# Router gates of tiles 0 to 7 as row sums on VectorE instead of turned rows and small matmuls on TensorE

## The reference, cut to what matters

```python
# _moe_ref: x is the attention output, (4, 576, 512)
u = x + real(fft(fft(x, axis=1), axis=2))
un = (u - mean(u)) / sqrt(var(u) + 1e-6)
x2 = u + maximum(un @ w_ch1, 0) @ w_ch2          # 512 -> 2048 -> 512
# _moe2_ref: 8 experts, 512 -> 1024 -> 512
logits = x2 @ w_gate                             # (512, 8)
local_gate = sigmoid(x2 @ w_local)               # (512, 1)
# position s takes argmax(logits) if s == 0 or local_gate < 0.5, else the expert of position s - 1
out[s] = softmax(logits)[e] * (maximum(x2[s] @ w1[e], 0) @ w2[e])
```

## Time and profile before

| | |
|---|---|
| median of 3 runs | 913.07 us (912.81 to 913.15) |
| the profiled execution, its own time | 915.11 us |
| its span, first to last instruction | 913.3 us |
| mean granted TensorE clock | 0.976 of full speed |
| TensorE busy | 859.9 us, 94% |
| VectorE busy | 460.6 us, 50% |
| ScalarE busy | 316.1 us, 35% |
| GpSimd busy | 272.5 us, 30% |

### The profile page before, as it was taken

One profiled execution on the slowest core, in us unless ns is written; L12 is line 12 of the kernel. 1 busy time (PEld: TensorE's weight loads), 2 busy tenths in 40 slices (PEclk: granted clock), 3 DMA queues, 4 the chain that ended last, 5 costly groups with the idle time before them and its releaser, 6 DMA issues.

```text
span 913.3 us, 22516 instructions
## 1 busy us (share of the span) xinstructions
PE 859.9 (94%) x9075; PEld 622.1 (68%) x9076; DVE 460.6 (50%) x852; ACT 316.1 (35%) x469; POOL 272.5 (30%) x287
## 2 busy tenths in 40 slices
PE   8988988899999999999999999929999999999995
PEld 4766767776767676767676767617777777777773
DVE  6889898857242424242424244658995884000000
ACT  5788887643111111111111111111333333333331
POOL 2457768311010101010101000002444444343331
PEclk9999999989999999999999999968999999999998
DMA  9454652455010101010101003504775772111110
GB/s 287 128 172 143 183 142 72 146 181 162 24 48 23 46 23 46 23 46 23 46 23 46 24 24 106 148 26 125 244 232 159 233 233 94 46 42 45 50 29 1
DMA packets 55675, 88.92 MB, mean 97 GB/s; under 512 B 7148, under 2 KB 26171, under 8 KB 55621
## 3 DMA queue, kind: packets, MB, share of 16 engines
q1 hardware_dynamic: 50261, 72.43, 25.7%
q0 software_dynamic: 5360, 15.74, 5.6%
HBM read 70.80 MB, written 16.55 MB: 96 GB/s over the span
## 4 chain that ended last, share of the span: by engine, by line
PE 77%; DVE 9%; DMA 5%; issue 3%; ACT 2%; SPq 2%; POOL 1%; DVEq 0%; POOLq 0%; ACTq 0%
PE psum L925 19%; PE psum L908 19%; PE psum L1089 14%; PE psum L1105 14%; DMA m_mem<-in_qk 2%; PE psum L660 2%; DVE m_mem L1416 1%; DMA arena<-in_mlp_w 1%; PE psum L1056 1%; DVE arena L1444 1%; PE psum L869 1%; DVE arena L1437 1%; DVE arena L1465 1%; PE psum L877 1%; PE psum L773 1%
## 5 line engine op out<-in xcount | busy, mean ns | idle before, releaser
L908 PE MATMUL psum<-m_mem,arena 128*128 (+1 forms) x1728 | 199.0, 273 | 0.0
L925 PE MATMUL psum<-arena,m_mem 128*128 128x512 f16 x864 | 195.3, 379 | 0.0
L908 PEld LDWEIGHTS psum<-m_mem,arena 128*128 128x128 f16 x1728 | 168.5, 98 | 25.9 <-issue 0.4
L925 PEld LDWEIGHTS psum<-arena,m_mem 128*128 128x128 f16 x864 | 84.5, 98 | 90.4
L1089 PEld LDWEIGHTS psum<-m_mem,arena 128*128 x2400 | 137.1, 97 | 7.0 <-issue 1.5
L1089 PE MATMUL psum<-m_mem,arena 128*128 128x128 f16 x2400 | 139.4, 218 | 1.3 <-issue 0.7
L1105 PE MATMUL psum<-arena,m_mem 128*128 x600 | 133.4, 379 | 0.0
L1272 ACT ACTIVATE m_mem<-psum 128x512 f16<-128x512 f32 x72 | 42.9, 596 | 242.4 <-PE psum L908 242.4
L1105 PEld LDWEIGHTS psum<-arena,m_mem 128*128 128x128 f16 x600 | 57.7, 98 | 65.2
L1598 DVE SCALAR_TENSOR_TENSOR m_mem<-psum,m_mem 128x512 f16<-128x512 f32 x72 | 49.7, 690 | 100.0 <-ACT m_mem L1272 99.9
L1994 POOL TENSOR_TENSOR arena<-m_mem,arena 128x1024 f16<-128x1024 f32 x9 | 18.0, 1996 | 270.1 <-ACT arena L1287 225.1
(11 more groups left out here) (242 smaller groups left out, 1071.7 us busy)
## 6 DMA issues: line engine op xcount, KB each, us to landing
dimdft_sb<-in_exp_w SPq DMA_DIRECT2D x74, 256.0 KB, 3.6
wstage<-in_exp_w SPq DMA_DIRECT2D x54, 256.0 KB, 3.0
m_mem<-in_qk SPq DMA_DIRECT2D x16, 576.0 KB, 4.8
arena<-in_v SPq DMA_DIRECT2D x32, 160.0 KB, 2.8
x_rows<-m_mem SPq DMA_DIRECT2D x16, 320.0 KB, 3.0
x_rows<-arena SPq DMA_DIRECT2D x9, 512.0 KB, 2.8
wstage<-in_mlp_w SPq DMA_DIRECT2D x16, 256.0 KB, 3.2
arena<-in_mlp_w SPq DMA_DIRECT2D x16, 256.0 KB, 3.6
```

Of the source, the lines that this page charges most:

```text
L908: last = nc.tensor.matmul(psum[:, 2 + k % 4, (f % 2) * 2 * P:(f % 2 + 1) * 2 * P], w1_sb[:, sp_, c, f * P:(f + 1) * P], unT[:, bass.ds(t % ...
L925: last = nc.tensor.matmul(psum[:, 6 + q, :], hT[:, k % 4, sp_, at:at + P], w2_sb[:, mp, f, :], start=f == 0 and sp_ == 0 and mp == 0, stop ...
```

## The change

The rows of x2 are not turned for tiles 0 to 7. For each of the nine gate columns and each half q, VectorE multiplies the 128x512 rows elementwise by the column, laid out as a row and repeated on all 128 partitions, and sums the products over the row into one word of `logits` per partition (`scalar_tensor_tensor` with an accumulator output). These are 18 instructions per tile, three behind `hidden_lo(0)` and five behind each of `hidden_lo(1)` to `hidden_lo(3)` of the following tile. The products themselves are written to a scratch space and not used.

The repeated columns are made ahead of tile 0: TensorE transposes the 128x36 gate matrix, VectorE copies it out, SyncE stores its 36 rows to memory and, behind the last MLP weight load, issues nine DMAs that read each column as a repeated source into 128 partitions (256 KB each). The last tile (t = 8) keeps the turned rows and the matmuls. The waits of `x2_of` and of the routing stage are changed to the new semaphore `gate_step`.

The diff, without its context lines:

```diff
@@ -120,6 +120,7 @@
+    gate_dram = nc.dram_tensor("gate_rows", [DC * (E + 1), P], F32).ap()
@@ -282,6 +283,12 @@
+        gate_at = [SLOT_WORDS, SLOT_WORDS + 2 * D] + [SLOT_WORDS - 2 * D * (i + 1) for i in range(5)]\
+            + [x_tail + 4 * D, x_tail + 6 * D]
+        gate_cols = [arena[:, at:at + 2 * D].bitcast(F32) for at in gate_at]
+        gateT = arena[0:DC * (E + 1), ends_at + 4 * D - 2 * P:ends_at + 4 * D].bitcast(F32)
+        assert ends_at + 4 * D <= min(gate_at)
+        products = [x288.bitcast(F16)[:, i * D:(i + 1) * D] for i in range(2)]
@@ -448,9 +455,11 @@
-        x2T_ready = sem("x2T_ready")
-        x2T_hi = sem("x2T_hi")
-        x2T_lo = sem("x2T_lo")
+        gateT_ready = sem("gateT_ready")
+        gateT_copied = sem("gateT_copied")
+        gate_out = sem("gate_out")
+        gate_in = sem("gate_in")
+        gate_step = sem("gate_step")
@@ -609,8 +618,15 @@
+            sp.wait_ge(gateT_copied, 1)
+            sp.dma_start(gate_dram, gateT).then_inc(gate_out, 16)
+            sp.wait_ge(gate_out, 16)
+            for e in range(E + 1):
+                sp.dma_start(gate_cols[e].rearrange("p (c j) -> p c j", c=DC),
+                             gate_dram.rearrange("(c e) j -> e c j", c=DC)[e].unsqueeze(0).to_broadcast([P, DC, P]))\
+                    .then_inc(gate_in, 16)
@@ -870,14 +886,6 @@
-            def transpose_x2(t):
-                pe.wait_ge(x2_done, t + 1)
-                for q in range(2):
-                    for c in range(DC):
-                        last = nc.tensor.transpose(psum[:, q, c * P:(c + 1) * P], x2_sb[:, q, c * P:(c + 1) * P],
-                                                   ident_sb[:, :])
-                last.then_inc(x2T_ready, 1)
             def gate_half(q):
@@ -886,13 +894,6 @@
-            def gate(t):
-                pe.wait_ge(x2T_lo, t + 1)
-                for q in range(2):
-                    last = gate_half(q)
-                last.then_inc(gate_ready, 1)
             def hidden(t, k, first):
@@ -930,17 +931,11 @@
             def mlp(t, first=False, last=False):
-                if not first:
-                    transpose_x2(t - 1)
-                if not first:
-                    gate(t - 1)
-                    if not first:
-                        pe.wait_ge(logits_done, t)
@@ -990,10 +985,11 @@
+            nc.tensor.transpose(psum[0:DC * (E + 1), 0, 0:P], wg_in.rearrange("p c e -> p (c e)"), ident_sb[:, :])\
+                .then_inc(gateT_ready, 1)
-            pe.wait_ge(wg_split, 1)
             with pe.Fori(1, MT - 1 - FIRST_TILE) as t:
@@ -1005,6 +1001,7 @@
+            pe.wait_ge(wg_split, 1)
@@ -1274,10 +1271,6 @@
-            def x2T_copy(t):
-                act.wait_ge(x2T_ready, t + 1)
-                nc.scalar.activation(x2T[:, 0], psum[:, 0:2, :], ACT.Copy).then_inc(x2T_hi, 1)
             def x2_hi_of(t, first=False):
@@ -1290,7 +1283,6 @@
-                    x2T_copy(t - 1)
@@ -1604,6 +1596,7 @@
+                    dve.wait_ge(gate_step, len(GATE_OPS) * t)
@@ -1613,12 +1606,23 @@
-            def x2T_lo_of(t):
-                dve.wait_ge(x2T_hi, t + 1)
-                nc.vector.tensor_tensor(x2T[:, 1], psum[:, 0:2, :], x2T[:, 0], ALU.subtract).then_inc(x2T_lo, 1)
+            GATE_OPS = [(q, e) for q in range(2) for e in range(E + 1)]
+            def gates_of(t, steps):
+                n = len(GATE_OPS)
+                dve.wait_ge(x2_done, t + 1)
+                for j in steps:
+                    if j > 1:
+                        dve.wait_ge(gate_step, n * t + j - 1)
+                    q, e = GATE_OPS[j]
+                    nc.vector.scalar_tensor_tensor(out=products[j % 2], in0=x2_sb[:, q, :], scalar=1.0 / XS, in1=gate_cols[e],
+                                                   op0=ALU.mult, op1=ALU.mult,
+                                                   accum_out=logits[:, q, bass.ds(tile_at(t), 1), e:e + 1]
+                                                   .rearrange("p o e -> p (o e)")).then_inc(gate_step, 1)
             def logits_of(t):
-                dve.wait_ge(gate_ready, t + 1)
+                dve.wait_ge(gate_ready, 1)
@@ -1642,10 +1646,8 @@
-                    if k == 1 and not first:
-                        x2T_lo_of(t - 1)
-                    if k == 2 and not first:
-                        logits_of(t - 1)
+                    if k < 4 and not first:
+                        gates_of(t - 1, range(5 * k - 2 if k else 0, 5 * k + 3))
@@ -1708,6 +1710,8 @@
+            dve.wait_ge(gateT_ready, 1)
+            nc.vector.tensor_copy(gateT, psum[0:DC * (E + 1), 0, 0:P]).then_inc(gateT_copied, 1)
@@ -1724,6 +1728,8 @@
+            dve.wait_ge(gate_in, 16 * (E + 1))
+            dve.wait_ge(edge_stored, 16)
             with dve.Fori(1, MT - 1) as t:
@@ -1758,7 +1764,8 @@
-            dve.wait_ge(logits_done, MT)
+            dve.wait_ge(gate_step, len(GATE_OPS) * (MT - 1))
+            dve.wait_ge(logits_done, 1)
```

## The result

| | before | after |
|---|---|---|
| median of the runs side by side | 912.94 us (912.04 to 913.15) | 901.12 us (899.51 to 903.43) |
| the profiled execution, its own time | 915.11 us | 899.51 us |
| its span | 913.3 us | 897.6 us |

The ratio is 0.9879, with an interval of 0.9854 to 0.9904: 1.2% faster, 11.8 us between the medians. 902.7 was predicted, with a range of 901.0 to 911.5.

The account below looks back on a forecast made before the run. TensorE was taken to bound tiles 1 to 8. Terms −12.0 + 0.55 + 0.5 + 0.6 = −10.35 us took the median from 913.07 to 902.7 us, range 901.0 to 911.5.

Parts of the forecast that it names:

- Removed from TensorE: Tiles 1 to 8: x2 transposes and gate matmuls go, saving 1.50 us a tile, 12.0 us in all.
- The step: VectorE: one multiply-and-sum of 128x512 costs 0.70 us, between 0.61 and 0.84; eighteen take 12.6 us.
- Rival B: VectorE's step runs at half rate, 0.51 us more each, making the kernel slower at 969 us; chance 0.09.
- GpSimd's meeting: Tiles 1 to 7: GpSimd's subtraction stretches one VectorE step per tile by 1.8 us.
- The slack ahead of the turned rows: Tiles 1 to 7: VectorE's normalised rows end 1.1 us before TensorE wants them for transpose_un.
- rival A: VectorE late for the turned rows: at 0.80 us a step, stalls of 0.7 us in seven tiles, 909 us; chance 0.18.
- The last tile: Tile 8: steps and weight splits make hidden_lo(4) late for TensorE, 0.6 us lost.
- Ahead of tile 0 and the chain to the turned rows: Gate-matrix transpose costs 0.2 us and SyncE's wait and store 0.35, so 0.55 us reach the end.
- The nine loads: Repeated-column loads on SyncE's queue: issues covered at 4.5 us, data at 270 GB/s nearly in time; 0.5 us taken.
- Rival C: Repeated loads run at half rate, a 7.5 us stall ahead of tile 0's last project, 910 us; chance 0.10.
- The forecast case: Whole kernel: median of 902.7 us, own range 901 to 905; chance 0.60.
- Rival D: TensorE's stream does not shorten because another wait fills the removed time, 913 us; chance 0.03.

Follow-up runs that it names:

- more8_shortpool: Changed kernel with eight further unused steps per tile in tiles 1 to 7 and GpSimd's subtraction cut from 128x1024 to 128x16: 910.76 us, ratio 0.9969.
- more8: Changed kernel with eight further unused multiply-and-sum steps per tile in tiles 1 to 7, ahead of the fold: 931.04 us, ratio 1.0178.
- best: Changed kernel with, in tile 0, the nine loads behind two expert chunks and hidden(0, 6) ahead of transpose_un(1): 898.35 us, ratio 0.9823.
- more4: Changed kernel with four further unused multiply-and-sum steps per tile in tiles 1 to 7, ahead of the fold: 903.33 us, ratio 0.9885.
- the second comparison: Changed kernel measured once more, with no further edit, against the kernel before: 901.59 us, ratio 0.9864.
- turn_back: Changed kernel with the eight x2 transposes put back on TensorE in tiles 1 to 8, result unused: 911.37 us, ratio 0.9973.
- loads_late: Changed kernel with the nine loads of repeated columns issued behind the first two expert chunks instead of ahead: 905.03 us, ratio 0.9919.

## Why the prediction was right

**Removed from TensorE, 12.0 us: right.** Eight tiles became shorter by 1.48 us each, 11.8 us. The other 0.02 us a tile is the edge of the reading. The transposes' share, 0.88 us, came back to the hundredth when they were put back.

**The step, 0.70 us: right in kind, 0.09 too high.** Two f32 sources from SBUF and a sum run as fast as the like of the earlier trace rows, 0.68 us; the write of the sum hides under the next instruction. My lower bound of 0.61 us was the value. The Trainium skill (VectorE: DVE Perf Modes, "Two Vector instructions with no wait between them") says that such an instruction is two; the trace agrees and adds the time, 0.08 us, and that the next step doesn't wait for it.

**Rival B and its rule: refuted.** The Trainium skill (Vector Engine (DVE) Microarchitecture Reference, "Points that are easy to get wrong") has the throughput of this instruction halved with two non-bf16 sources in SBUF. Here the one with a sum takes 0.68 us and the one without 0.69 us: the rule does not hold for it.

**GpSimd's meeting, 1.8 us, one step per tile: right in tiles 1 to 7.** 2.48 instead of 0.68 us, and gone when GpSimd's piece was cut. In tile 8 it met a weight split (545.23, 2.37 us) instead of a step. The Trainium skill (SBUF — State Buffer, "Who interferes with whom") says that a VectorE instruction with two SBUF inputs contends with a GpSimd instruction that reads SBUF, and that the pair of ports they share is an exclusive lock. The rows fit that: GpSimd's piece runs from 236.23 to 238.38, and the step that began at 236.46 ends at 238.94, 0.56 us behind it.

**The slack ahead of the turned rows, 1.1 us: mis-sized, on the safe side.** The fold starts at 248.02 and the normalised rows end at 254.06, where TensorE takes them at 256.79: 2.7 us (2.3 in tile 7). Of the 1.6 us between, 1.45 are the fold's earlier start (18.85 us into the tile instead of 20.3): the step's 0.09 us times 18, less 0.18 us that VectorE stands still ahead of `hidden_lo(1)`. The rest is the way from the fold to the rows, 6.04 instead of 6.2 us. The experiments bracket it: 2.44 us more fit in tiles 1 to 6 and miss by 0.2 in tile 7, 4.9 us more stall TensorE by 2.1. Where rival A begins stays as predicted, 0.61 + 2.7 / 18 = 0.76 us a step; the step stayed far below. At the 0.7 us that rival A named its price was nearly right: stalls of 0.8 us made a tile 1.0 us longer in `more8_shortpool`. Further on it was too low: stalls of 2.1 us cost 1.6 more by the clock in most tiles, which neither the rival nor the range had in it.

**The last tile, 0.6 us lost: wrong, nothing lost.** This too is the step's price: `hidden_lo(4)` starts at 564.88, ends at 565.56, and TensorE takes it at 566.52.

```profile
564.88 0.68 DVE L1590 SCALAR_TENSOR_TENSOR m_mem<-psum,m_mem 128x512 f16<-128x512 f32 x1
...
566.52 2.75 PE L926 MATMUL psum<-arena,m_mem 128*128 128x512 f16 x12
```

I had it 1.6 us later, 18 x 0.09 once more. The 5.92 us wait for a load was filled by steps as predicted; no split of tile 8 waits for a DMA any more.

**Ahead of tile 0 and the chain to the turned rows, 0.55 us: 0.2 seen, the rest not.** From the transposes ahead of the edge matmuls to tile 0's start the kernel before took 5.43 and 5.44 us; `more8` and `best`, with the new transpose and equally slow turning transposes (1.97 us), took 5.65 both: 0.21 us more, the 0.2 of the sum. Whether it reaches the end, the scatter hides. From tile 0's start to the turned rows the kernel before took 29.8 and 30.3 us, the changed one 29.4 and 29.7. The scatter is as large as the 0.35 us for SyncE's queue; that part can be neither confirmed nor excluded.

**The nine loads, 0.5 us: right in place, but the working was wrong.** I counted their issues at 4.5 us, covered. They take 9.69 us, and they, not the data rate, were under-priced: the window 213 to 219 us of the changed kernel moved 304 GB/s, above the 270 I had used, so a repeated source is not slow. Rival C's size falls (a stall of 7.5 us), but its sign came in a small form: VectorE waited 5.63 us for the expert chunk, and TensorE was idle ahead of the last `project`, for 0.41 us in the first profile and 1.81 us in the second (1.50 in `more4`, 1.12 in `more8_shortpool`). The first agrees with my 0.5 by luck, out of two errors of opposite sign. In the three profiles with the loads in this place in which the clock fell in tile 0, the idle time ahead of the last `project` was gone, and the tile took 48.0 to 48.4 us, against 46.55 to 48.20 without a fall: the one delay hides the other.

**Sum.** −11.8 in tiles 1 to 8 and the idle 0.4 to 1.8 us ahead of the last `project` would give −10.0 to −11.4, where −10.35 was predicted; the medians say −11.8 and, in the second comparison, 901.59 − 913.48 = −11.9. So tile 0 as a whole did not grow by what its new wait suggests: it took 46.31 and 48.49 us before, 46.55 and 48.20 after. The forecast case was the one that came. It ended 1.6 us above the time: the 0.6, the 0.55 and the 0.5 do not show in the medians, less the 0.2 by which the removed work was too high. Rival D needed TensorE to find another wait: it has none in tiles 1 to 8.

## What to carry to other kernels

Where one engine fills its window to the last tenth, the saving of removing work from it is its start-to-start distance in the trace, times the count, and this came out within 2% of itself, 1.48 us a tile against 1.50. The work that moves to another engine is free as long as its last due result is in time, so the sum to make is the slack at each due point, step by step, with every meeting of GpSimd and a two-source VectorE instruction in it; and when the slack is short, a stall of 2 us should be priced at up to 4 us (a tile of 48.15 instead of 44.09 us). A stage with a scattered wait (tile 0) hides gains of 1 us and is best repaired by giving the waiting engine other work first.

## What was not expected of the hardware

**TensorE's clock after a short idle time.** After an idle time of about 2 us the granted clock often, but not always, fell from 2.4 to 1.2 GHz for a few microseconds, and cost 1.6 to 1.7 us on top of the wait. In the tiles 0 of all profiles, the idle times ahead of the turned rows of 1.99, 2.02, 2.22, 2.38 and 2.44 us were followed by slow matmuls, those of 1.50, 1.70, 1.77 and 1.89 us and one of 2.21 us were not. In the kernel with eight extra steps equal idle times of 2.16 us went both ways. In the experts, 2.08 us of idle time was followed by a window at 0.63 (`turn_back`), 1.59 us by one at 1.00 (`loads_late`). What decides between them is open.

**The time before tile 0 scatters.** With the same instructions, tile 0 began between 182.62 and 186.78 us in the profiled executions, while the tile period of each kernel was the same to 0.01 us wherever VectorE was in time. A change in the tiles should be read from the period, not from one median.
